# Rounded-and-rest products for the tokens' mean squares, and an earlier softmax division, in a fused attention and feed-forward kernel

## The chip, the cores and the metric

The kernel runs on one core of one Trainium2 chip. The metric is device time in microseconds (us) of one execution. The comparison is between the kernel before and the same kernel with the change below.

## What is computed

The reference has three stages, in float32.

```python
# attention, per batch (8) and head (8); 576 tokens, head width 64, 32 packing rows
p_packed = softmax(p k^T / 8) v          # first softmax, 32 rows
out      = softmax(q p_packed^T / 8) p_packed   # second softmax, 576 rows of 32 entries
x = out, heads side by side              # 4608 tokens x 512
# first feed-forward, inner width 1536
rms = sqrt(mean(x * x) + 1e-6)           # one number per token
xn  = x / rms * rms_g
x   = (silu(xn @ w_gate) * (xn @ w_val)) @ w_out
# second feed-forward
out = ((x @ w1) * (x @ w2)) @ w3 @ w_out2
```

## The kernel before, in words

**The attention is never multiplied out.** Per batch, the second softmax gives weights a2 of 32 entries per head and token. The kernel folds `p_packed`, the gain and `w_gate`/`w_val` into small matrices M (item "M" below), so that the first feed-forward's inner product is M against a2. The tokens' mean squares come from the same weights: with G the 32x32 inner products of a head's packed rows, a token's sum of squares is the sum over heads of a2^T G a2. G stands on the diagonal of two 128x128 matrices, the tile `gram` (one for even heads, one for odd: "parities"). Item "Z" multiplies `gram` by a2 on TensorE (L782); VectorE multiplies that by a2 again (L1363); GpSimd adds the parities (L648); item "SS" transposes and VectorE sums (L1368); GpSimd takes the power -0.5 (L655); after a trip through DRAM a2 is scaled by the result (L662), and a2 is split for the next batch's products.

**Rounded parts and rests.** The large products are done as three products of type fp32r: with a value x cut to x_hi (rounded, written as fp32r) and x_lo = x - x_hi, the product is hi hi + hi lo + lo hi, summed in PSUM. ScalarE (ACT) makes the hi parts and VectorE (DVE) the lo parts. The small items (S1, S2, G, Z, M, and transposes) take plain fp32 operands.

**The slots.** The main loop has 8 batches of 24 slots. A slot n handles one chunk of 128 inner columns for half the batch's tokens (288). TensorE (PE) issues in slot n:

- `into`: 12 fp32r products of 288 columns (L853 to L855), six for gate, six for val. The gate part waits for `u_ready` of slot n-1, the val part for `h_ready` of slot n-1, since they rewrite those PSUM banks (0 and 1);
- `outof`: 6 fp32r products of 512 columns (L877 to L879) from the chunk two slots earlier. It waits for `hl_ready` of the chunk;
- then the items that a table written out by hand, `SLOT_ITEMS`, puts behind this slot. They prepare the next batch (or, for S1, the one after).

ACT in slot n: the evictions of the items of slot n-1; exp1/exp2 where due; tanh of the gate part (L1262, waits for `gate_done`); the rounding of h into `g_hx` (L1269, "cast", waits for h); in even slots the issue of a small DMA (`store_rest`, L1243). DVE in slot n: the evictions of the items of slot n-1; `g_s` (L1566, waits for tanh), then `u_ready`; `g_h` (L1572), then `h_ready`; steps of the second softmax where due; "hl", the rest of h (L1587, waits for the cast), then `hl_ready`; further steps where due. Each engine takes its instructions strictly in the order written, so a wait holds all that is behind it.

The items around the change:

```python
SLOT_ITEMS = {..., 13: [("S2", 1, 1), ("M", 1, 0)], 14: [("Z", 1, 0)],
              15: [("S1", 2, 0), ("M", 1, 1)], 17: [("Z", 1, 1)], 18: [("SS", 1, 0)], ...}
```

Some items ("on gate": the first item of a slot that has two, so S2 in slot 13 and S1 in slot 15) use banks 0 and 1, the banks of gate and val. Before such an item PE waits for `u_ready` and `h_ready` of this very slot, and the next slot's gate part waits until the first half of the item has been evicted (for S2: the transposition L1357, on DVE, signal `s2_half`).

```python
for it in slot_items(n - 1):
    if on_gate(it) and it[0] in ("S1", "S2") and which == 0:
        pe.wait_ge((s1_half, s2_half)[it[0] == "S2"], 2 * it[1] + it[2] + 1)
```

The steps of the second softmax, for the two halves of the tokens (part 0 and 1): `shift2` (L1411, L1413) in slots 9 and 14; exp2 (L1131, ACT) in 11 and 15; `sums2` (L1419, L1421, L1423) in 11 and 15, behind hl; `normalize2` (L1428 and the transposition into `a2T`, L1434) in 13 and 16, between g_h and hl; `inner` writes `gram` (L1388) in slot 10; Z in 14 and 17. The S2 of part 1 writes over `a2`, so L1357 waits for the `a2T` of part 0.

Of the kernel before, what the change touches and what calls it, by code (L numbers as in the profile page):

```python
# [5 lines left out]
ALU = mybir.AluOpType  # L6
ACT = mybir.ActivationFunctionType
AX = mybir.AxisListType
F32 = mybir.dt.float32
F32R = mybir.dt.float32r  # L10

P = 128
# [51 lines left out]


SHIFT1, EXP1, SUMS1 = 21, (0, 3), 4
SHIFT2, EXP2, SUMS2, NORM2 = (9, 14), (11, 15), (11, 15), (13, 16)
GRAM = 10

REST_AHEAD = (0, 3)  # L70
WARM = 7
# [66 lines left out]
def build(nc, kT_d, qT_d, v_d, pT_d, g_d, w_gate, w_val, w_o, w12, w3T, w_out, out, r_dram, y_dram, wf_dram, rest_dram, w12_dram):  # L138
    ctx = ExitStack()
    with ctx:  # L140
        def sem(name):
            return ctx.enter_context(nc.semaphore(name))
# [21 lines left out]
        with ExitStack() as st:  # L164
            at = alloc(st)
            w_in = [at(f"w_in{i}", [P, KC, BANK]) for i in range(W_BUFS)]
            kT = at("kT", [P, HC, S])
            qT = [at(f"qT{i}", [P, HC, HALF]) for i in range(2)]
            v_sb = at("v_sb", [P, BLOCKS, HC * DH])
            pT = at("pT", [P, HC * NP])  # L170
            sc = at("sc", [P, 2, S])
            a1T = at("a1T", [P, BLOCKS * P])
            pp = at("pp", [P, 2 * DH])
            ppT = at("ppT", [P, P])
            ppTg = at("ppTg", [P, P])
            gc, gram = at("gc", [P, 2, NP]), at("gram", [P, 2, P])
            a2 = at("a2", [P, 2, HALF])
            wz = at("wz", [P, 2, HALF])
            wsum = at("wsum", [P, S])
            r_sb = at("r_sb", [P, S])  # L180
            a2T = at("a2T", [P, 2, 2, HALF])

            g_s, g_h = at("g_s", [P, HALF]), at("g_h", [P, HALF])
        w_raw, w_lo, w_hi = [None] * PAIRS, [None] * PAIRS, [None] * PAIRS

        def raw_and_lo(stack, name, shape):
# [138 lines left out]
        xy_full, xy_free = sem("xy_full"), sem("xy_free")  # L325
        nmax1_ready, bias1_ready, e1_ready = sem("nmax1_ready"), sem("bias1_ready"), sem("e1_ready")
        den1_ready, rden1_ready = sem("den1_ready"), sem("rden1_ready")
        gram_ready, s1_half, s2_half = sem("gram_ready"), sem("s1_half"), sem("s2_half")
        ppg_ready, ssum_ready, msum_ready = sem("ppg_ready"), sem("ssum_ready"), sem("msum_ready")
        max2_ready, d2_ready, e2_ready, sum2_ready = sem("max2_ready"), sem("d2_ready"), sem("e2_ready"), sem("sum2_ready")  # L330
# [37 lines left out]
        def full(eng, kind, a, part):  # L368

            eng.wait_ge(xy_full, number[kind, a, part] + 1)  # L370
# [354 lines left out]
        def _(pe):  # L725
            def item(kind, a, part):
# [44 lines left out]
                if kind == "S2":  # L771
                    freed(pe, "PT", a, 0)
                    pe.wait_ge(q_loaded[part], 16 * (a + 1))
                    for c in range(HC):
                        for par in range(2):
                            rows, cols = slice(DH * par, DH * (par + 1)), slice(NP * c, NP * (c + 1))
                            last = nc.tensor.matmul(xy[par][cols, 0:HALF], ppT[rows, cols], qT[part][rows, c, :], start=True, stop=True)
                if kind == "Z":
                    pe.wait_ge(gram_ready, a + 1)
                    pe.wait_ge(a2T_ready, 2 * a + part + 1)  # L780
                    for par in range(2):
                        last = nc.tensor.matmul(xy[par][:, 0:HALF], gram[:, par, :], a2T[:, part, par, :], start=True, stop=True)  # L782
# [303 lines left out]
        def _(act):  # L1086
# [42 lines left out]
            def exp2(a, t):  # L1129
                act.wait_ge(d2_ready, 2 * a + t + 1)  # L1130
                nc.scalar.activation(a2[:], a2[:], ACT.Exp, scale=SCALE).then_inc(e2_ready, 1)  # L1131

            def a2_split(a, t):
                act.wait_ge(a2s_ready, 2 * a + t + 1)
                if a:

                    act.wait_ge(val_done, SLOTS * a - 1 + t)
                nc.scalar.copy(a2_hi[:, t, :, :], a2T[:, t, :, :]).then_inc(a2hi_ready, 1)
# [8 lines left out]
            def wo_split(f):  # L1147
                act.wait_ge(wo_loaded[next(i for i, rows in enumerate(WO_LOADS) if f < rows.stop)], 16)
                nc.scalar.copy(wo_hi[:, f, :], wo_raw[:, f, :]).then_inc(wo_hi_ready, 1)
# [95 lines left out]
            for n in range(LAST):  # L1245
                b, s = divmod(n, SLOTS)
                f, t = divmod(s, 2)
                k = n // 2
                if s == 1 and b > 0:
                    evict(b - 1, (0, 1))  # L1250
                if s == 2 and b > 0:
                    evict(b - 1, (2,))
                for it in slot_items(n - 1):
                    item(*it)
                if b + 1 < B and s in EXP1 and n:
                    exp1(b + 1, EXP1.index(s))
                if b + 1 < B and s in EXP2:
                    exp2(b + 1, EXP2.index(s))
                act.wait_ge(gate_done, n + 1)
                if n:  # L1260
                    act.wait_ge(h_ready, n)
                nc.scalar.activation(g_s[:], in_ps[0], ACT.Tanh, scale=0.5).then_inc(s_ready, 1)  # L1262
                if n == 1:
                    wo_split(0)
                act.wait_ge(h_ready, n + 1)
                if t == 1 and k >= 2:

                    act.wait_ge(rest_stored[k % 2], 16 * (k // 2))
                nc.scalar.copy(g_hx[f % 2][:, 0, HALF * t:HALF * (t + 1)], g_h[:]).then_inc(hh_ready, 1)  # L1269
                if 0 < n < SLOTS and t == 0:  # L1270
                    wo_split(f)
                if b + 1 < B and s >= SLOTS - 2:
                    a2_split(b + 1, t)
                if t == 0 and k >= 1:
                    store_rest(k - 1)
# [73 lines left out]
        def _(dve):  # L1349
# [75 lines left out]
            def normalize2(a, t):  # L1425
                k = 2 * a + t
                dve.wait_ge(rden2_ready, k + 1)
                nc.vector.tensor_tensor(heads(a2[:]), heads(a2[:]), rden2[:].unsqueeze(2).to_broadcast([P, GROUPS2, NP]),  # L1428
                                        ALU.mult).then_inc(a2_ready, 1)
                dve.wait_ge(a2_ready, k + 1)  # L1430
                if a:

                    dve.wait_ge(a2lo_ready, k - 1)
                nc.vector.transpose(a2T[:, t, :, :], a2[:]).then_inc(a2T_ready, 1)  # L1434

            def a2_split(a, t):
                dve.wait_ge(a2hi_ready, 2 * a + t + 1)
                nc.vector.tensor_tensor(a2_lo[:, t, :, :], a2T[:, t, :, :], a2_hi[:, t, :, :].bitcast(F32),
                                        ALU.subtract).then_inc(a2lo_ready, 1)
# [116 lines left out]
            for n in range(LAST):  # L1556
                b, s = divmod(n, SLOTS)
                f, t = divmod(s, 2)
                if s == 2 and b > 0:
                    evict(b - 1)  # L1560
                behind = [it for it in slot_items(n - 1) if it[0] == "M" and it[2] not in REST_AHEAD]
                for it in slot_items(n - 1):
                    if it not in behind:
                        item(*it)
                dve.wait_ge(s_ready, n + 1)
                nc.vector.scalar_tensor_tensor(out=g_s[:], in0=g_s[:], scalar=1.0, in1=in_ps[0],  # L1566
                                               op0=ALU.add, op1=ALU.mult).then_inc(u_ready, 1)
                dve.wait_ge(u_ready, n + 1)
                dve.wait_ge(val_done, n + 1)
                if n:  # L1570
                    dve.wait_ge(hl_ready, n)
                nc.vector.scalar_tensor_tensor(out=g_h[:], in0=g_s[:], scalar=0.5, in1=in_ps[1],  # L1572
                                               op0=ALU.mult, op1=ALU.mult).then_inc(h_ready, 1)
                if n == 1:
                    wo_split(0)
                if b + 1 < B and s == SUMS1:
                    sums1(b + 1)
                if b + 1 < B and s in SHIFT2:
                    shift2(b + 1, SHIFT2.index(s))
                if b + 1 < B and s in NORM2:  # L1580
                    normalize2(b + 1, NORM2.index(s))
                for it in behind:
                    if n > 1:
                        item(*it)
                dve.wait_ge(hh_ready, n + 1)
                own = slice(HALF * t, HALF * (t + 1))
                nc.vector.tensor_tensor(g_hx[f % 2][:, 1, own], g_h[:], g_hx[f % 2][:, 0, own].bitcast(F32),  # L1587
                                        ALU.subtract).then_inc(hl_ready, 1)
                if n == 1:

                    item("M", 0, 2)
                if 0 < n < SLOTS and t == 0:
                    wo_split(f)
                if b + 2 < B and s == SHIFT1:
                    shift1(b + 2)
                if b + 1 < B and s == GRAM:
                    inner(b + 1)
                if b + 1 < B and s in SUMS2:
                    sums2(b + 1, SUMS2.index(s))
                if b + 1 < B and s >= SLOTS - 2:  # L1600
                    a2_split(b + 1, t)
            for c in range(FC):
# [152 lines left out]
```

## Time and profile before

| what | value |
|---|---|
| median of 3 runs | 1320.36 us (1319.73 to 1320.95) |
| the profiled execution: its own time | 1319.28 us |
| the profiled execution: span, first to last instruction | 1317.7 us |
| PE busy | 1311.3 us, 100% of the span |
| DVE busy | 874.2 us, 66% |
| ACT busy | 411.8 us, 31% |
| POOL busy | 122.4 us, 9% |
| chain that ended last | PE 98%, DVE 1% |
| main loop of 192 slots | from 61.2 us to about 736 us |

The busy share of PE is of records that overlap: a product of 288 columns shows 0.29 us, while the next one starts 0.13 us after it. What a product costs is read from start to start. "PEld" rows are weight loads, which run beside the product before. On DVE and ACT too an instruction can start up to 0.1 us before the one ahead is shown as ended, when nothing makes it wait. A timeline row has the start, the duration, the engine, the line and operation, output and inputs with their shapes, and in brackets the idle time before it with the engine that ended the idle time.

### The profile page before, as it was taken

The numbers are of one execution on the slowest core, as the hardware profiler recorded it, in microseconds if no ns is written. First come the engines' busy times: TensorE is split into PE (matmuls) and PEld (weight loads), VectorE is DVE, ScalarE is ACT, GpSimd is POOL, SyncE is SP. The second block draws the span as 40 slices with busy tenths as digits, with TensorE's granted clock in tenths as the row PEclk, the third lists the DMA queues.
The fourth block names the chain that finished last, engine by engine and source line by source line (L and its number), as shares of the span: only waits on it lengthen the run. The fifth ranks groups of instructions, "written<-read, shape, count | busy, mean of one in ns | idle before, by whom it ended". The sixth has DMA issues, their size and how long they took to land.

```text
span 1317.7 us, 21671 instructions
## 1 busy us (share of the span) xinstructions
PE 1311.3 (100%) x8590; PEld 1089.4 (83%) x8590; DVE 874.2 (66%) x1373; ACT 411.8 (31%) x787; POOL 122.4 (9%) x92
## 2 busy tenths in 40 slices
PE   9999999999999999999999999999999999999998
PEld 7788878888878888887888899888888888888887
DVE  5668667576565765756754677866766686677666
ACT  5344433434434344343333433311200120112000
POOL 0100101001000010010100531100200010020000
PEclk9999999999999999999999999999999999999999
DMA  9773435343534434333426386845454335545301
GB/s 356 245 271 121 158 123 168 127 160 108 173 97 159 167 118 162 125 120 104 114 77 234 139 312 264 308 142 183 128 176 160 128 117 195 179 147 188 101 1 64
DMA packets 117202, 211.40 MB, mean 160 GB/s; under 512 B 33904, under 2 KB 35952, under 8 KB 114032
## 3 DMA queue, kind: packets, MB, share of 16 engines
q1 hardware_dynamic: 90672, 203.21, 45.0%
q10 hardware_dynamic: 26432, 6.82, 2.3%
q8 instruction: 69, 1.13, 0.4%
q14 instruction: 29, 0.24, 0.1%
HBM read 168.04 MB, written 41.96 MB: 159 GB/s over the span
## 4 chain that ended last, share of the span: by engine, by line
PE 98%; DVE 1%; ACT 0%; DMA 0%; issue 0%; SPq 0%; ACTq 0%
PE psum L965 9%; PE psum L967 9%; PE psum L966 9%; PE psum L853 8%; PE psum L855 8%; PE psum L854 8%; PE psum L879 7%; PE psum L878 7%; PE psum L877 7%; PE psum L1008 4%; PE psum L1010 4%; PE psum L1009 4%; PE psum L798 3%; PE psum L819 1%; PE psum L782 1%; PE psum L824 1%
## 5 line engine op out<-in xcount | busy, mean ns | idle before, releaser
L853 PE MATMUL psum<-a_hi,m_hi 128*128 128x288 f32 x768 | 235.2, 306 | 1.2 <-DVE g_s L1566 0.4
L855 PE MATMUL psum<-a_hi,m_lo 128*128 128x288 f32 x768 | 226.4, 295 | 0.0
L854 PE MATMUL psum<-a_lo,m_hi 128*128 128x288 f32 x768 | 226.2, 295 | 0.0
L853 PEld LDWEIGHTS psum<-a_hi,m_hi 128*128 128x128 f32 x768 | 144.2, 188 | 47.1 <-issue 39.6
L1566 DVE SCALAR_TENSOR_TENSOR g_s<-g_s,psum 128x288 f32<-128x288 f32 x192 | 86.6, 451 | 129.7 <-ACT g_s L1262 129.1
L879 PE MATMUL psum<-g_hx,wo_lo 128*128 128x512 f32 x384 | 152.3, 397 | 0.0
L878 PE MATMUL psum<-g_hx,wo_hi 128*128 128x512 f32 x384 | 151.6, 395 | 0.0
L1269 ACT CAST g_hx<-g_h 128x288 fp32r<-128x288 f32 x192 | 83.1, 433 | 218.5 <-DVE g_h L1572 215.5
L877 PE MATMUL psum<-g_hx,wo_hi 128*128 128x512 f32 x384 | 150.3, 391 | 0.0
L854 PEld LDWEIGHTS psum<-a_lo,m_hi 128*128 128x128 f32 x768 | 144.4, 188 | 5.2
L855 PEld LDWEIGHTS psum<-a_hi,m_lo 128*128 128x128 f32 x768 | 144.1, 188 | 0.0
L1587 DVE TENSOR_TENSOR g_hx<-g_h,g_hx 128x288 fp32r<-128x288 f32 x192 | 90.2, 470 | 68.6 <-ACT g_hx L1269 68.6
L1340 ACT CAST hhd<-hd_raw 128x1024 fp32r<-128x1024 f32 x15 | 15.8, 1054 | 295.7 <-DVE hd_raw L1680 286.8
L1262 ACT ACTIVATE g_s<-psum 128x288 f32<-128x288 f32 x192 | 78.9, 411 | 93.1 <-PE psum L855 91.6
L1008 PE MATMUL psum<-wf_hi,hhd 128*128 128x512 f32 x256 | 100.4, 392 | 0.1
L1010 PE MATMUL psum<-wf_hi,hd_lo 128*128 128x512 f32 x256 | 99.7, 389 | 0.0
L1009 PE MATMUL psum<-wf_lo,hhd 128*128 128x512 f32 x256 | 99.7, 389 | 0.0
L1514 DVE TENSOR_TENSOR bd<-bd,psum 128x512 f32<-128x512 f32 x96 | 65.8, 687 | 41.1 <-PE psum L1010 39.9
L1572 DVE SCALAR_TENSOR_TENSOR g_h<-g_s,psum 128x288 f32<-128x288 f32 x192 | 87.1, 454 | 6.9 <-DVE g_s L1566 0.3
L965 PE MATMUL psum<-xd_hi,w_hi 128*128 128x512 f32 x224 | 87.2, 389 | 0.0
L966 PE MATMUL psum<-xd_lo,w_hi 128*128 128x512 f32 x224 | 87.2, 389 | 0.0
L967 PE MATMUL psum<-xd_hi,w_lo 128*128 128x512 f32 x224 | 87.1, 389 | 0.0
(188 smaller groups left out, 2413.9 us busy)
## 6 DMA issues: line engine op xcount, KB each, us to landing
w_in<-in_w_gate SPq DMA_DIRECT2D x24, 1024.0 KB, 7.3
w_in<-in_w_val SPq DMA_DIRECT2D x24, 1024.0 KB, 5.2
wb_hi<-w_scratch SPq DMA_DIRECT2D x56, 256.0 KB, 2.8
wb_lo<-w_scratch SPq DMA_DIRECT2D x56, 256.0 KB, 3.1
w_hi<-w_scratch SPq DMA_DIRECT2D x49, 256.0 KB, 3.0
w_lo<-w_scratch SPq DMA_DIRECT2D x49, 256.0 KB, 3.9
kT<-in_kT SPq DMA_DIRECT2D x8, 1152.0 KB, 7.2
v_sb<-in_v SPq DMA_DIRECT2D x8, 1152.0 KB, 9.9
```

The source lines that it names most:

```text
L853: nc.tensor.matmul(in_ps[which], hi, a2_hi[:, t, par, :], start=par == 0, stop=False)
L854: nc.tensor.matmul(in_ps[which], hi, a2_lo[:, t, par, :], start=False, stop=False)
L855: last = nc.tensor.matmul(in_ps[which], lo, a2_hi[:, t, par, :], start=False, stop=par == 1)
L877: nc.tensor.matmul(out_ps[m], hi, hh, start=f == 0, stop=False)
L878: nc.tensor.matmul(out_ps[m], hi, hl, start=False, stop=False)
L879: last = nc.tensor.matmul(out_ps[m], lo, hh, start=False, stop=f == FC - 1)
L965: nc.tensor.matmul(dst, hi, xhi[:, c, :], start=c == 0, stop=False)
L966: nc.tensor.matmul(dst, hi, xlo[:, c, :], start=False, stop=False)
L967: last = nc.tensor.matmul(dst, lo, xhi[:, c, :], start=False, stop=c == 1)
L1008: nc.tensor.matmul(dst, hhd[:, f, cols], wf_hi[:, chunk, :], start=f == 1, stop=False)
L1009: nc.tensor.matmul(dst, hhd[:, f, cols], wf_lo[:, chunk, :], start=False, stop=False)
L1010: last = nc.tensor.matmul(dst, hld[:, f, cols], wf_hi[:, chunk, :], start=False, stop=f == 0)
```

## The change

The Z of batches 1 to 7 no longer multiplies `gram` by `a2T` in fp32, but takes three fp32r products per parity from four new tiles: `gram_hi`, `gram_lo`, `z_hi`, `z_lo`. Batch 0, whose preparation is ahead of the loop, keeps the fp32 products. ACT makes `gram_hi` in slot 11 and `z_hi` in slots 12 and 16, each behind the slot's cast; DVE makes `gram_lo` in slot 11, behind hl and ahead of `sums2`, and `z_lo` in slots 13 and 16, as the last step of the slot. `normalize2` of part 0 goes from slot 13 to slot 12 (same place, between g_h and hl); that of part 1 goes from slot 16, between g_h and hl, to slot 15, behind `sums2`. Z stays in slots 14 and 17.

```diff
-SHIFT2, EXP2, SUMS2, NORM2 = (9, 14), (11, 15), (11, 15), (13, 16)
+SHIFT2, EXP2, SUMS2, NORM2 = (9, 14), (11, 15), (11, 15), 12
 GRAM = 10
+GRAM_SPLIT, Z_HI, Z_LO = 11, (12, 16), (13, 16)
...
+            gram_hi, gram_lo = at("gram_hi", [P, 2, P], F32R), at("gram_lo", [P, 2, P], F32R)
+            z_hi, z_lo = at("z_hi", [P, 2, HALF], F32R), at("z_lo", [P, 2, HALF], F32R)
...
-                if kind == "Z":
+                if kind == "Z" and a:
+                    pe.wait_ge(z_lo_ready, 3 * (a - 1) + part + 2)
+                    for par in range(2):
+                        nc.tensor.matmul(xy[par][:, 0:HALF], gram_hi[:, par, :], z_hi[:, par, :], start=True, stop=False)
+                        nc.tensor.matmul(xy[par][:, 0:HALF], gram_hi[:, par, :], z_lo[:, par, :], start=False, stop=False)
+                        last = nc.tensor.matmul(xy[par][:, 0:HALF], gram_lo[:, par, :], z_hi[:, par, :], start=False, stop=True)
+                if kind == "Z" and a == 0:
                     pe.wait_ge(gram_ready, a + 1)
                     pe.wait_ge(a2T_ready, 2 * a + part + 1)
...
(ACT)
+            def gram_split(a):
+                act.wait_ge(gram_ready, a + 1)
+                if a > 1:
+                    full(act, "Z", a - 1, 1)
+                nc.scalar.copy(gram_hi[:], gram[:]).then_inc(z_hi_ready, 1)
+            def z_split(a, t):
+                act.wait_ge(a2T_ready, 2 * a + t + 1)
+                if t:
+                    full(act, "Z", a, 0)
+                nc.scalar.copy(z_hi[:], a2T[:, t, :, :]).then_inc(z_hi_ready, 1)
...
                 nc.scalar.copy(g_hx[f % 2][:, 0, HALF * t:HALF * (t + 1)], g_h[:]).then_inc(hh_ready, 1)
                 if 0 < n < SLOTS and t == 0:
                     wo_split(f)
+                if b + 1 < B and s == GRAM_SPLIT:
+                    gram_split(b + 1)
+                if b + 1 < B and s in Z_HI:
+                    z_split(b + 1, Z_HI.index(s))
...
(DVE)
+            def gram_split(a):
+                dve.wait_ge(z_hi_ready, 3 * (a - 1) + 1)
+                if a > 1:
+                    full(dve, "Z", a - 1, 1)
+                nc.vector.tensor_tensor(gram_lo[:], gram[:], gram_hi[:].bitcast(F32), ALU.subtract).then_inc(z_lo_ready, 1)
+            def z_split(a, t):
+                dve.wait_ge(z_hi_ready, 3 * (a - 1) + t + 2)
+                if t:
+                    full(dve, "Z", a, 0)
+                nc.vector.tensor_tensor(z_lo[:], a2T[:, t, :, :], z_hi[:].bitcast(F32), ALU.subtract).then_inc(z_lo_ready, 1)
...
-                if b + 1 < B and s in NORM2:
-                    normalize2(b + 1, NORM2.index(s))
+                if b + 1 < B and s == NORM2:
+                    normalize2(b + 1, 0)
...
                 if b + 1 < B and s == GRAM:
                     inner(b + 1)
+                if b + 1 < B and s == GRAM_SPLIT:
+                    gram_split(b + 1)
                 if b + 1 < B and s in SUMS2:
                     sums2(b + 1, SUMS2.index(s))
+                if b + 1 < B and s == SUMS2[1]:
+                    normalize2(b + 1, 1)
+                if b + 1 < B and s in Z_LO:
+                    z_split(b + 1, Z_LO.index(s))
                 if b + 1 < B and s >= SLOTS - 2:
                     a2_split(b + 1, t)
```

## Rows read from the trace of the kernel before

**Rows 1.** The page: the chain that ended last, by engine.

```profile
PE 98%; DVE 1%; ACT 0%; DMA 0%; issue 0%; SPq 0%; ACTq 0%
```

**Rows 2.** Timeline of PE: end of slot 11, start of slot 12.

```profile
188.81 0.40 PE L879 MATMUL psum<-g_hx,wo_lo 128*128 128x512 f32 x1
189.04 0.29 PE L853 MATMUL psum<-a_hi,m_hi 128*128 128x288 f32 x1
189.17 0.29 PE L854 MATMUL psum<-a_lo,m_hi 128*128 128x288 f32 x1
```

**Rows 3.** Timeline of PE: end of slot 14 with its Z, start of slot 15.

```profile
199.59 0.40 PE L879 MATMUL psum<-g_hx,wo_lo 128*128 128x512 f32 x1
199.82 1.14 PE L782 MATMUL psum<-a2T,gram 128*128 128x288 f32 x4
...
200.92 0.29 PE L854 MATMUL psum<-a_lo,m_hi 128*128 128x288 f32 x1
```

**Rows 4.** Instructions on the tile a2T (ns min/median/max): the subtraction for a2_lo.

```profile
L1438 DVE TENSOR_TENSOR a_lo<-a2T,a_hi x16: 754/759/1272, 58.8 to 661.7; 128x576 fp32r<-128x576 f32 x16
```

**Rows 5.** Timeline of PE: end of slot 13, its items, start of slot 14.

```profile
194.77 0.40 PE L879 MATMUL psum<-g_hx,wo_lo 128*128 128x512 f32 x1
195.09 0.71 PE L777 MATMUL psum<-qT,ppT 64*32 64x288 f32 x16
195.60 1.06 PE L798 MATMUL psum<-w_in,ppTg 64*32 64x512 f32 x16
196.76 0.37 PE L853 MATMUL psum<-a_hi,m_hi 128*128 128x288 f32 x1
196.97 0.29 PE L854 MATMUL psum<-a_lo,m_hi 128*128 128x288 f32 x1
```

**Rows 6.** Timeline of PE: M of slot 15, start of slot 16.

```profile
204.38 1.06 PE L798 MATMUL psum<-w_in,ppTg 64*32 64x512 f32 x16
...
205.61 0.30 PE L854 MATMUL psum<-a_lo,m_hi 128*128 128x288 f32 x1
```

**Rows 7.** Timeline of DVE: hl of slot 11 to the eviction of S2 in slot 14.

```profile
188.94 0.46 DVE L1587 TENSOR_TENSOR g_hx<-g_h,g_hx 128x288 fp32r<-128x288 f32 x1 [0.50 <-ACT g_hx L1269]
189.31 0.75 DVE L1419 TENSOR_REDUCE sum<-a 128x18 f32<-128x576 f32 x1
...
190.49 0.44 DVE L1566 SCALAR_TENSOR_TENSOR g_s<-g_s,psum 128x288 f32<-128x288 f32 x1
190.96 0.45 DVE L1572 SCALAR_TENSOR_TENSOR g_h<-g_s,psum 128x288 f32<-128x288 f32 x1
191.92 0.46 DVE L1587 TENSOR_TENSOR g_hx<-g_h,g_hx 128x288 fp32r<-128x288 f32 x1 [0.50 <-ACT g_hx L1269]
193.45 0.46 DVE L1566 SCALAR_TENSOR_TENSOR g_s<-g_s,psum 128x288 f32<-128x288 f32 x1 [1.08 <-ACT g_s L1262]
...
194.31 0.75 DVE L1428 TENSOR_TENSOR a<-a,rden 128x576 f32<-128x576 f32 x1
195.10 0.78 DVE L1434 STREAM_TRANSPOSE a2T<-a 128x576 f32<-128x576 f32 x1
...
196.14 0.47 DVE L1357 STREAM_TRANSPOSE a<-psum 128x288 f32<-128x288 f32 x1
```

**Rows 8.** Timeline of ACT: cast of slot 11, tanh of slot 13; then slot 23.

```profile
188.47 0.43 ACT L1269 CAST g_hx<-g_h 128x288 fp32r<-128x288 f32 x1 [1.01 <-DVE g_h L1572]
...
193.01 0.41 ACT L1262 ACTIVATE g_s<-psum 128x288 f32<-128x288 f32 x1 [1.12 <-PE psum L855]
...
232.80 0.67 ACT L1138 CAST a_hi<-a2T 128x576 fp32r<-128x576 f32 x1
233.38 0.20 ACT L1122 ACTIVATE bias<-nmax 128x2 f32<-128x2 f32 x1
```

**Rows 9.** Timeline of DVE: hl of slot 15, g_s of slot 16.

```profile
203.84 0.46 DVE L1587 TENSOR_TENSOR g_hx<-g_h,g_hx 128x288 fp32r<-128x288 f32 x1 [0.50 <-ACT g_hx L1269]
...
206.91 0.45 DVE L1566 SCALAR_TENSOR_TENSOR g_s<-g_s,psum 128x288 f32<-128x288 f32 x1 [1.44 <-ACT g_s L1262]
```

More of the change, by code:

```diff
@@ L327, in build @@
         den1_ready, rden1_ready = sem("den1_ready"), sem("rden1_ready")
+        z_hi_ready, z_lo_ready = sem("z_hi_ready"), sem("z_lo_ready")
         gram_ready, s1_half, s2_half = sem("gram_ready"), sem("s1_half"), sem("s2_half")
```

## The prediction, made before the changed kernel ran

> **What bounds the kernel now.** I read the page first. TensorE (PE) is busy for the whole span, and the chain that ended last is PE for 98% of it [rows 1]. So work on ACT or DVE costs nothing while it stays beside PE, and every stop of PE is paid in full. The question is what PE saves in Z, and whether what ACT and DVE get to do makes PE wait. The second view is therefore PE's timeline, start to start, since the records overlap. Without items, the last `outof` product of a slot starts at 188.81 and the second `into` product of the next slot at 189.17, 0.36 us later; the first begins the slot at 189.04 [rows 2]. The third view is the timelines of DVE and ACT in slots 11 to 16, read for how much time lies between the moment a signal is given and the moment PE wants it. All times below are of one batch; the slots repeat in the others.
>
> One place is already tight. From the start of M in slot 13 to the second product of slot 14 it is 196.97 - 195.60 = 1.37 us [rows 5]; behind the M of slot 15 it is 205.61 - 204.38 = 1.23 [rows 6]. The missing 0.14 us is a wait: slot 14's gate part needs S2's first half evicted, and that transposition starts at 196.14 [rows 7], 0.62 us ahead of PE's product at 196.76 [rows 5]. DVE, not PE, sets the start of slot 14 now, and whatever makes DVE later there makes the kernel longer.
>
> **What Z gives back.** With Z between, the last `outof` product and the second `into` product are 200.92 - 199.59 = 1.33 us apart [rows 3], against 0.36 without: Z costs 0.97 us. After the change it is six fp32r products of 288 columns, like those of `into`. The first product of slot 12 starts 0.23 us after the last `outof` one and the second 0.13 later [rows 2]. So six cost 0.13 to 0.133 each, 0.80 us at most, and the gain is 0.17 to 0.18 us for each Z. Changed are 7 batches of two parts: 14 x 0.175 = 2.45 us. A Z is recorded as four instructions [rows 3], two for each of its two fp32 products, at 0.97 / 4 = 0.24 each. Bounds per Z: nothing gained if products from the new tiles step more slowly than in `into`, 0.24 gained if each of the six took half of such a record.
>
> Rows give 0.97 for two fp32 products, 0.24 per record. The Trainium skill, page FP8 and Floating Point Precision, section TensorE Precision Notes, says that true fp32 takes four passes through the array; three passes against four would be a quarter of 0.97 saved, 0.24 per Z and 3.4 us in all, an estimate by that page. The trace agrees only in part: fp32r products step at 0.13 [rows 2], not at 0.12, a quarter of one fp32 product.
>
> **What the moves cost: the chain into slot 14.** I follow it from hl of slot 11, start 188.94, which the change leaves where it is.
>
> - ACT: `gram_hi` starts behind the cast of slot 11 (188.47 [rows 8]), at about 188.8, and lasts under 0.43, what the cast of 288 columns takes. DVE's `gram_lo` can start at about 189.3, where hl leaves DVE free (188.94 to 189.31 [rows 7]). For 256 columns it holds DVE about 0.34, a little under hl's 0.37.
> - `sums2` therefore starts at 189.65, not 189.31. It holds DVE for 1.18 (189.31 to 190.49), so g_s of slot 12 starts at 190.82, g_h 0.47 later (190.49 to 190.96) at 191.29. PE wants them at about 192.0 and 192.8 (slot 12 began at 189.04 [rows 2]; a slot without items is 12 x 0.13 + 6 x 0.23, about 3.0): no stop here.
> - New in slot 12: `normalize2`. It starts 0.37 after g_h, at 191.66; its transposition 0.79 later (194.31 to 195.10 [rows 7]), at 192.45, takes 0.78.
> - ACT waits for that: `z_hi` at about 193.26, 0.03 after the transposition ends, as g_s starts 0.03 after tanh ends (193.01 + 0.41 to 193.45 [rows 7, 8]). Behind it on ACT stands tanh of slot 13, which ran at 193.01 before [rows 8]. A rounding of this size lets the next ACT instruction start 0.58 later (232.80 to 233.38 [rows 8]): tanh at 193.84. The DMA that ACT issues in slot 12 stands behind `z_hi` as well, goes out beside it about 1.8 us later than now, and its data is first read after the loop. tanh is 0.83 late.
> - g_s of slot 13 follows tanh by 0.44 (193.01 to 193.45 [rows 7]): 194.28. g_h 0.48 later, 194.77, ends at 195.22. S2, which started at 195.09 [rows 5], waits for it: it starts about 0.2 late. hl follows g_h by 0.96 (190.96 to 191.92): 195.73.
> - New in slot 13: `z_lo` of part 0, at 196.10. The same subtraction takes 0.76 [rows 4] and, like hl, lets the next start 0.08 or 0.09 before its end: 0.67 to 0.68. S2's eviction starts at 196.77 or 196.78 instead of 196.14.
> - PE follows 0.62 later, at 197.40 instead of 196.76.
>
> Slot 14 starts 0.64 us late, S2's own lateness included. That `normalize2` left slot 13 gives DVE 1.49 us there, but the wait on tanh, `gram_lo` and `z_lo` take more. **Bounds of this stop.** Low: 0.57, if S2's eviction counts from its end by the shortest hand-over of these rows (0.03 after the end of a 0.47 us instruction, and as much for PE's load) instead of the 0.62. High: 0.80, if the new hand-over of `a2T` and one other show the tail of 0.15 that PE shows behind S2's eviction (0.62 - 0.47). I take 0.64, to which every step has a row of its own kind.
>
> **Is anything else late?** M's eviction, shift2 and exp2 move with PE. Slot 15 starts 0.64 - 0.17 = 0.47 late. There DVE gets `normalize2` of part 1 behind `sums2`. hl of slot 15, 203.84 before [rows 9], comes at about 204.2 to 204.3; `sums2` 1.18 and the division and transposition (about 0.1 of own wait, 0.79, and 0.78 less the usual 0.08) end at about 207.4. g_s of slot 16 was at 206.91 [rows 9] and would be at 207.4 with PE: DVE is free just as it is due, and PE wants that signal only at the start of slot 17, over 1 us later. In slot 16 1.49 us leave DVE and 0.67 (`z_lo`) come. `z_hi` of part 1 finds its input ready. In slot 17 Z finds `z_lo` over 1 us old, and in slot 14 over 3 us. Hidden at no price: `gram_hi`, `z_hi` of part 1, `z_lo` of part 1. If PE did not lead there, `z_lo` would cost its 0.67 us per batch. No step on POOL or on SP's queue is moved; what they wait for (Z's eviction, M's products) moves with PE.
>
> **The sum.** Per batch: 0.64 lost in slot 13, 2 x 0.175 = 0.35 saved: 0.29 us longer. Seven batches: +2.0 us. The profiled execution took 1319.28 us (span 1317.7), so it would take 1321.3. That execution is 1.1 below the median 1320.36 of the runs; against the median the forecast is 1322.4 us, +0.15%. A difference under 0.2%, 2.6 us, is about what a measurement of this kernel can't tell from none.
>
> **Rivals.**
>
> 1. *The chain hands over more slowly (slower).* Place: `a2T` to `z_hi` to tanh of slot 13. The trace has no engine waiting for `a2T` at once. For: PE's product came 0.15 behind the end of S2's transposition. Against: the one hand-over from ACT to DVE in the rows takes 0.03. It decides slower if the stop passes 0.35 + 0.38 = 0.73 us per batch. At 0.8 to 0.9 it is +3.1 to +3.9 us: 1323.5 to 1324.3. Chance 0.22.
> 2. *The chain is not binding (only the gain).* `z_hi` would have to cost tanh nothing. For: PE stands well ahead of DVE elsewhere. Against: slot 14 already starts on S2's eviction [rows 5 to 7]; `z_lo` alone, put ahead of it, is 0.67. It gives 1320.4 - 2.4 = 1317.9. Chance 0.08.
> 3. *Z becomes no cheaper.* If the weights of six short products are not hidden here, Z takes 0.97 as before (the change then doesn't do what it says) and only the stop is left: 7 x 0.64 = +4.5, 1324.9. Against: `into` loads the same kind of weights beside products of the same width. Chance 0.05.
> 4. *A second stop in slots 16 or 17*, where DVE is just free at 207.4. It must be over 0.6 us late to reach PE; then 0.1 to 0.4 us per batch on top, 1323.1 to 1325.2. Chance 0.07.
>
> The forecast has the rest, 0.58. With the gain per Z from 0.15 to 0.20 and the stop from 0.57 to 0.75, it goes from +1.2 to +3.2: 1321.5 to 1323.6.
>
> **How the numbers follow.** Of the forecast's 0.58 about 0.13 lies above +2.6 us; with rival 1 (0.19 of it), rival 3 (0.05) and rival 4 (0.06) slower has 0.43. Rival 2 straddles -2.6 us and gives faster 0.04; two more hundredths go to a gain near the page's figure together with it: 0.06. The rest, 0.51, is no change. The range holds the forecast, rival 1 and rival 4 and leaves out most of rivals 2 and 3: 1319.8 to 1325.6, with 0.6 us of the runs' own spread at either end.
>
> **What would show it.** In the changed profile: Z as six products at 0.13, the distance of 1.33 become 1.16. `z_hi` of slot 12 starts right after `a2T`, and tanh of slot 13 right after `z_hi`, released by ACT's own order and not by PE. S2's eviction behind `z_lo`, and from the last `outof` product of slot 13 to the start of slot 14 about 2.6 us in place of 196.76 - 194.77 = 1.99 [rows 5], with PE idle ahead of S2 and ahead of slot 14. No new idle time on PE in slots 15 to 18. I am wrong if slot 13 is not longer, if tanh of slot 13 still starts 1.0 us into its slot, or if another slot has grown.

## The result, and the profile after

| kernel | median | runs |
|---|---|---|
| before | 1320.95 us (1319.18 to 1321.94) | 9 |
| changed | 1323.25 us (1322.65 to 1324.57) | 9 |

The ratio is 1.0022, with a 95% interval of 1.0014 to 1.0030: 1.8 to 4.0 us slower, where 2.0 was forecast; the two medians are 2.3 us apart. The profiled execution of the changed kernel took 1322.82 us, with a span of 1321.2 and a granted clock of 1.000.

The chain that ended last, by engine (page of the changed kernel; compare [rows 1]):

```profile
PE 93%; DVE 4%; ACT 1%; issue 1%; POOL 0%; ACTq 0%; POOLq 0%
```

DVE and ACT now hold 5% of the chain between them; before it was 1% [rows 1]. The waits of PE and of its weight loads say where (engine and line waited for: us in total, times, longest; two views of the changed kernel):

```profile
PE psum L865 <- DVE a L1385: 3.4, 7, 0.5
```

```profile
PEld psum L783 <- DVE g_s L1606: 4.4, 7, 0.9
```

L865 is the first gate product of a slot, L1385 the eviction of S2, L783 S2 itself: seven waits of each kind, one per batch. The second view puts S2's wait down to the line of g_s; the g_h behind it is the later of the two signals that S2 waits for.

Timeline of PE in the changed kernel, the same batch as [rows 5] (the whole batch lies 0.9 us later): the end of slot 13, S2, M and the start of slot 14.

```profile
195.68 0.40 PE L891 MATMUL psum<-g_hx,wo_lo 128*128 128x512 f32 x1
196.25 0.72 PE L783 MATMUL psum<-qT,ppT 64*32 64x288 f32 x16 [0.17 <-issue]
196.73 1.09 PE L810 MATMUL psum<-w_in,ppTg 64*32 64x512 f32 x16
198.31 0.37 PE L865 MATMUL psum<-a_hi,m_hi 128*128 128x288 f32 x1 [0.48 <-DVE a L1385]
```

From the last `outof` product to slot 14 it is 198.31 - 195.68 = 2.63 us, against 1.99 before; "about 2.6" was forecast. S2 starts 0.57 behind that product in place of 0.32, and slot 14 starts 1.58 behind M in place of 1.16.

The chain behind that, on DVE, hl of slot 11 to S2's eviction (compare [rows 7]):

```profile
189.85 0.46 DVE L1627 TENSOR_TENSOR g_hx<-g_h,g_hx 128x288 fp32r<-128x288 f32 x1 [0.50 <-ACT g_hx L1293]
190.23 0.42 DVE L1468 TENSOR_TENSOR gram_lo<-gram,gram_hi 128x256 fp32r<-128x256 f32 x1
190.56 0.75 DVE L1447 TENSOR_REDUCE sum<-a 128x18 f32<-128x576 f32 x1
...
191.74 0.40 DVE L1606 SCALAR_TENSOR_TENSOR g_s<-g_s,psum 128x288 f32<-128x288 f32 x1
192.17 0.45 DVE L1612 SCALAR_TENSOR_TENSOR g_h<-g_s,psum 128x288 f32<-128x288 f32 x1
192.54 0.75 DVE L1456 TENSOR_TENSOR a<-a,rden 128x576 f32<-128x576 f32 x1
193.32 0.78 DVE L1462 STREAM_TRANSPOSE a2T<-a 128x576 f32<-128x576 f32 x1
194.03 0.41 DVE L1627 TENSOR_TENSOR g_hx<-g_h,g_hx 128x288 fp32r<-128x288 f32 x1
195.21 0.45 DVE L1606 SCALAR_TENSOR_TENSOR g_s<-g_s,psum 128x288 f32<-128x288 f32 x1 [0.77 <-ACT g_s L1286]
195.69 0.45 DVE L1612 SCALAR_TENSOR_TENSOR g_h<-g_s,psum 128x288 f32<-128x288 f32 x1
196.65 0.46 DVE L1627 TENSOR_TENSOR g_hx<-g_h,g_hx 128x288 fp32r<-128x288 f32 x1 [0.50 <-ACT g_hx L1293]
197.02 0.75 DVE L1474 TENSOR_TENSOR z_lo<-a2T,z_hi 128x576 fp32r<-128x576 f32 x1
197.69 0.47 DVE L1385 STREAM_TRANSPOSE a<-psum 128x288 f32<-128x288 f32 x1
```

and on ACT, `gram_hi` in slot 11, then `z_hi` and tanh of slot 13 (compare [rows 8]):

```profile
189.72 0.40 ACT L1149 CAST gram_hi<-gram 128x256 fp32r<-128x256 f32 x1
190.94 0.41 ACT L1286 ACTIVATE g_s<-psum 128x288 f32<-128x288 f32 x1 [0.82 <-PE psum L867]
192.65 0.43 ACT L1293 CAST g_hx<-g_h 128x288 fp32r<-128x288 f32 x1 [1.30 <-DVE g_h L1612]
194.13 0.67 ACT L1155 CAST z_hi<-a2T 128x576 fp32r<-128x576 f32 x1 [1.05 <-DVE a2T L1462]
194.14 0.52 ACTq L1267 DMA_DIRECT2D rest_scratch<-g_hx  x1
194.76 0.41 ACT L1286 ACTIVATE g_s<-psum 128x288 f32<-128x288 f32 x1
```

ACT's `z_hi` waits for `a2T` (L1462), with the DMA issue beside it, and tanh of slot 13 starts only at 194.76, 1.82 us into a slot that began at 192.94; it was 0.99 before. From hl of slot 11 to S2's eviction 7.84 us pass; before it was 196.14 - 188.94 = 7.20.

Z in slot 14, with the products around it (compare [rows 3]):

```profile
201.14 0.40 PE L891 MATMUL psum<-g_hx,wo_lo 128*128 128x512 f32 x1
201.38 0.29 PE L787 MATMUL psum<-z_hi,gram_hi 128*128 128x288 f32 x1
201.51 0.29 PE L788 MATMUL psum<-z_lo,gram_hi 128*128 128x288 f32 x1
201.64 0.29 PE L789 MATMUL psum<-z_hi,gram_lo 128*128 128x288 f32 x1
201.77 0.29 PE L787 MATMUL psum<-z_hi,gram_hi 128*128 128x288 f32 x1
201.90 0.30 PE L788 MATMUL psum<-z_lo,gram_hi 128*128 128x288 f32 x1
202.03 0.29 PE L789 MATMUL psum<-z_hi,gram_lo 128*128 128x288 f32 x1
202.16 0.29 PE L865 MATMUL psum<-a_hi,m_hi 128*128 128x288 f32 x1
202.30 0.29 PE L866 MATMUL psum<-a_lo,m_hi 128*128 128x288 f32 x1
```

Last `outof` product to second `into` product: 202.30 - 201.14 = 1.16 us, against 1.33. Z costs 0.80 in place of 0.97.

The start of one slot to the start of the next, read off PE's timeline for every batch, gives the whole account. All slots not listed are equal within 0.1 us, but for slots 22, 23 and 0 of some batches and slot 2 of batch 0, of which more below. Slots 14 and 15, and 17 and 18, stand together because a slot's first product is recorded 0.34 us ahead of the second behind the fp32 Z (200.58 and 200.92 in the kernel before) and 0.14 ahead behind the fp32r Z (202.16 and 202.30): the border between two slots moves, their sum doesn't.

| slots | before, batches 0 to 6 | changed, batches 1 to 6 | changed, batch 0 |
|---|---|---|---|
| 13 (S2, M) | 4.73 to 4.74 | 5.37 to 5.38 | 5.69 |
| 14 and 15 (Z; S1, M) | 8.61 (8.69 in batch 0, 8.13 in 6) | 8.44 (7.96 in 6) | 8.43 |
| 17 and 18 (Z; SS) | 7.51 (7.48 in batch 6) | 7.34 | 7.34 |

### The profile page after: what moved, and what is told of

The parts are those of the page before. It is cut to its first block, busy times and chain, and to the rows that moved or that the text cites. A ratio compares the mean times of both kernels' runs of the same rounds, so it can differ in the third digit from the quotient of the medians.

```text
span 1321.2 us, 21795 instructions
## 1 busy us (share of the span) xinstructions
PE 1310.8 (99%) x8618; PEld 1090.9 (83%) x8618; DVE 887.7 (67%) x1394; ACT 422.3 (32%) x808; POOL 121.5 (9%) x92
## 4 chain that ended last, share of the span: by engine, by line
PE 93%; DVE 4%; ACT 1%; issue 1%; POOL 0%; ACTq 0%; POOLq 0%
PE psum L977 9%; PE psum L979 9%; PE psum L978 9%; PE psum L865 8%; PE psum L867 7%; PE psum L866 7%; PE psum L891 6%; PE psum L890 6%; PE psum L889 6%; PE psum L1020 4%; PE psum L1022 4%; PE psum L1021 4%; PE psum L810 3%; PE psum L831 1%; PE psum L836 1%; PE psum L841 1%
## 5 line engine op out<-in xcount | busy, mean ns | idle before, releaser
L865 PE MATMUL psum<-a_hi,m_hi 128*128 128x288 f32 x768 | 232.8, 303 | 3.8 <-DVE a L1385 3.4
L865 PEld LDWEIGHTS psum<-a_hi,m_hi 128*128 128x128 f32 x768 | 144.2, 188 | 49.7 <-issue 43.0
L1627 DVE TENSOR_TENSOR g_hx<-g_h,g_hx 128x288 fp32r<-128x288 f32 x192 | 91.5, 477 | 68.3 <-ACT g_hx L1293 68.3
```

Source lines behind the costliest of these rows:

```text
L865: nc.tensor.matmul(in_ps[which], hi, a2_hi[:, t, par, :], start=par == 0, stop=False)
```

## The experiments

Distances of slots are read as in the table above. Medians and ratios are against the kernel before, run beside each on the same chip.

**1. The division alone.** The kernel before, with only this changed:

```diff
-SHIFT2, EXP2, SUMS2, NORM2 = (9, 14), (11, 15), (11, 15), (13, 16)
+SHIFT2, EXP2, SUMS2, NORM2 = (9, 14), (11, 15), (11, 15), 12
...
-                if b + 1 < B and s in NORM2:
-                    normalize2(b + 1, NORM2.index(s))
+                if b + 1 < B and s == NORM2:
+                    normalize2(b + 1, 0)
...
+                if b + 1 < B and s == SUMS2[1]:
+                    normalize2(b + 1, 1)
```

> The kernel before with only the two divisions moved (slot 13 to 12, slot 16 to behind the sums of slot 15); Z stays fp32, no splits. Theory (tanh of slot 13 is late only because z_hi stands before it and waits for a2T; z_lo stands before S2's eviction): nothing waits for the earlier division, DVE is free earlier in slot 13, so S2's eviction starts as soon as PE is through with S2, and slot 13 shrinks from 4.74 to about 4.6 us; 7 x 0.15 = 1.0 us faster than before, about 1319.9. Rival A (the moved division itself makes DVE late): slot 13 grows by up to 0.64, +4.5 us.

Measured: 1319.42 us against 1320.72, ratio 0.9990 (0.9981 to 0.9999). Slot 13 is 4.57 to 4.58 in all seven batches. Rival A falls: the earlier division by itself takes away what slot 14 already waited for S2's eviction. From the start of slot 13 to the second product of slot 14 it is 4.81 us in place of 4.95, so the wait was 0.14; the first product alone shows 0.16, since without a wait it is recorded 0.24 ahead of the second and with one 0.21. (The same 0.03 stands in slot 13 of experiments 3 and 6.) The stop comes from the splits around it.

**2. The stop without the gain.** The changed kernel with `gram` and `a2T` in Z again, splits and waits kept:

```diff
                     pe.wait_ge(z_lo_ready, 3 * (a - 1) + part + 2)
                     for par in range(2):
-                        nc.tensor.matmul(xy[par][:, 0:HALF], gram_hi[:, par, :], z_hi[:, par, :], start=True, stop=False)
-                        nc.tensor.matmul(xy[par][:, 0:HALF], gram_hi[:, par, :], z_lo[:, par, :], start=False, stop=False)
-                        last = nc.tensor.matmul(xy[par][:, 0:HALF], gram_lo[:, par, :], z_hi[:, par, :], start=False, stop=True)
+                        last = nc.tensor.matmul(xy[par][:, 0:HALF], gram[:, par, :], a2T[:, part, par, :], start=True, stop=True)
```

> The changed kernel with all splits and waits kept, but Z of every batch in fp32 from gram and a2T. Isolates the cost of the stop from the gain. Theory: slot 13 stays at 5.38, each of 14 Z costs 0.97 again in place of 0.80: 2.4 us slower than the changed kernel, 4.8 us slower than before (0.36%). Rival B (fp32r products gain nothing net, since PE only waits elsewhere for what it saved): no slower than the changed kernel, within 0.5 us.

Measured: 1325.05 us against 1320.72, ratio 1.0033 (1.0020 to 1.0045), 4.3 us slower. Slot 13 is 5.37 to 5.38 (5.68 in batch 0), slots 14 and 15 together 8.60, slots 17 and 18 together 7.51. The distances show stop and gain independent of each other: 14 x 0.17 = 2.4 us are lost again, as forecast, and the loops of the two profiles are 2.6 us apart. The medians of the time show less: those of this kernel and of the changed one are 1.8 us apart, were measured on different occasions, and the intervals of the two ratios overlap, so the time alone doesn't settle the size of the gain. Rival B, which allowed 0.5, falls by the distances.

**3. `z_lo` of part 0 behind S2's eviction.**

```diff
-GRAM_SPLIT, Z_HI, Z_LO = 11, (12, 16), (13, 16)
+GRAM_SPLIT, Z_HI, Z_LO = 11, (12, 16), (None, 16)
...
                     if it not in behind:
                         item(*it)
+                    if it[0] == "S2" and it[2] == 1:
+                        z_split(it[1], 0)
```

> The changed kernel with z_lo of part 0 put in slot 14 between the evictions of S2 and M, where DVE waits for M's rounding anyway. Theory: S2's eviction starts 0.67 earlier, then M's own products set the start of slot 14, 0.99 after M's start; slot 13 about 4.78 in place of 5.38; 7 x 0.6 = 4.2 us faster than the changed kernel, 2.1 faster than before. Rival C (the tanh of slot 13 is the only thing that matters, z_lo has slack): no change to the changed kernel.

Measured: 1320.07 us against 1320.72, ratio 0.9999 (0.9990 to 1.0008): about 3 us faster than the changed kernel (ratios 0.9999 and 1.0022, forecast 4.2), but not the 2.1 faster than before: the interval of the time reaches from 1.3 us faster to 1.1 slower. Slot 13 is 4.82 (5.13 in batch 0). The 0.56 us came back, so rival C falls; what stays, 0.25 above the 4.57 of experiment 1, is S2's own wait for the late g_h. The rest of the miss is batch 0 (0.3 in slot 13; 0.4 in slot 15, for which see experiment 6; 0.4 in slots 1 to 3, which stays open) and 0.9 us in slots 22, 23 and 0 around the ends of batches 1 and 2 in the profiled execution.

**4. `z_hi` of part 0 behind the cast of slot 13**, `z_lo` where the change has it:

```diff
-GRAM_SPLIT, Z_HI, Z_LO = 11, (12, 16), (13, 16)
+GRAM_SPLIT, Z_HI, Z_LO = 11, (13, 16), (13, 16)
```

> The changed kernel with only z_hi of part 0 moved from slot 12 to slot 13, behind the cast; z_lo stays at the end of slot 13, ahead of S2's eviction. Theory: tanh of slot 13 is on time (1.0 us into its slot), z_lo starts when z_hi is through, S2's eviction 0.62 earlier than in the changed kernel; slot 13 about 4.75; 4.3 us faster than the changed kernel, 2.1 to 2.4 faster than before. If instead the delay of tanh cost nothing: slot 13 stays at 5.38.

Measured: 1319.53 us against 1321.29, ratio 0.9986 (0.9977 to 0.9995). That is 1.8 us faster than before (0.7 to 3.0) where 2.1 to 2.4 was forecast. Slot 13 is 4.74 to 4.76 in batches 1 to 6, as forecast. In batch 0 it is 5.64, and only 0.05 came back: DVE splits `wo` in slot 12 as well, so g_s of slot 13 comes only 0.23 us earlier behind hl of slot 11, though tanh is on time; and `z_lo`, which stood 0.38 behind hl of slot 13, stands 0.57 behind it, since `z_hi` now waits for the cast.

**5. `gram_lo` one slot later:**

```diff
-                if b + 1 < B and s == GRAM_SPLIT:
+                if b + 1 < B and s == GRAM_SPLIT + 1:
                     gram_split(b + 1)
                 if b + 1 < B and s in SUMS2:
```

> The changed kernel with gram_lo moved from slot 11, ahead of the sums, to slot 12 behind hl. Theory: the whole chain (sums, g_s, g_h, division, transposition, z_hi, tanh) comes 0.33 earlier: slot 13 about 5.05 in place of 5.38, 2.3 us faster than the changed kernel, the time of the kernel before. If gram_lo was hidden: no change.

Measured: 1321.73 us against 1321.29, ratio 1.0000 (0.9990 to 1.0010). Slot 13 is 5.10 to 5.11 in five of seven batches (5.48 in batch 0; 5.39 in batch 2, where DVE stood 0.31 us between g_s and g_h of slot 12 for a reason that stays open; the kernel before has the same pause once, in slot 11 of batch 3). `gram_lo`'s 0.33 us was 0.27 of the stop.

**6. Both splits of part 0 late** (the edits of experiments 3 and 4, with `Z_HI, Z_LO = (13, 16), (None, 16)`):

> As z_lo_late, and z_hi of part 0 put in slot 13 behind the cast, so that tanh of slot 13 no longer waits for it. Theory: PE meets no wait in slot 13; 4.6 us in place of 5.38 (and of 4.74 before); Z keeps its gain: 3.4 to 3.5 us faster than before (0.26%), 5.8 faster than the changed kernel. Rival D (more work on ACT and DVE costs as such, wherever it stands): at most half of that.

Measured: 1318.14 us against 1320.72, ratio 0.9982 (0.9974 to 0.9991). Slot 13 is 4.57 to 4.58 (4.87 in batch 0), slots 14 and 15 together 8.46, slots 17 and 18 together 7.34. DVE and PE there, two views of this kernel:

```profile
196.21 0.48 DVE L1385 STREAM_TRANSPOSE a<-psum 128x288 f32<-128x288 f32 x1 [0.56 <-PE psum L783]
196.61 0.44 DVE L1386 STREAM_TRANSPOSE a<-psum 128x288 f32<-128x288 f32 x1
196.98 0.71 DVE L1474 TENSOR_TENSOR z_lo<-a2T,z_hi 128x576 fp32r<-128x576 f32 x1
198.11 1.23 DVE L1407 TENSOR_TENSOR m_lo<-psum,m_hi 128x1024 fp32r<-128x1024 f32 x1 [0.42 <-ACT m_hi L1127]
```

```profile
195.38 0.72 PE L783 MATMUL psum<-qT,ppT 64*32 64x288 f32 x16
195.89 1.06 PE L810 MATMUL psum<-w_in,ppTg 64*32 64x512 f32 x16
196.88 0.40 PE L865 MATMUL psum<-a_hi,m_hi 128*128 128x288 f32 x1
```

S2's eviction waits for PE (0.56 us idle, put down to L783), not PE for it; `z_lo` stands in time in which DVE waits for M's rounding, and 0.42 of that is still idle. This version is faster than both kernels: 2.6 us less than before, 5.1 less than the changed one, by medians measured on different occasions. The forecast was 3.4 to 3.5. Of the miss 0.3 us lie in slot 13 of batch 0 and 0.4 in its slot 15 (4.96 in place of 4.59), which is a stop at another place: in batch 0 DVE has a split of `wo` (L1492) in slot 14 too, works without a pause from 113.31 to 117.69, and g_s of slot 15 is the last of that work. S1 waits for g_s and g_h (DVE, then the weight loads of PE):

```profile
115.98 0.69 DVE L1492 TENSOR_TENSOR wo_lo<-wo_raw,wo_hi 128x512 fp32r<-128x512 f32 x1
...
117.25 0.44 DVE L1608 SCALAR_TENSOR_TENSOR g_s<-g_s,psum 128x288 f32<-128x288 f32 x1
```

```profile
118.25 0.21 PEld L743 LDWEIGHTS psum<-kT,pT 64*32 64x32 f32 x16 [0.71 <-DVE g_s L1608]
```

In the later batches no S1 waits for DVE. Rival D allowed 1.75 us at most; the interval of the time reaches from 1.2 to 3.4 us and doesn't exclude that by itself, but the distances do: in batches 1 to 6 slots 13 to 18 keep the whole gain, and all else that is lost there is 0.2 us around the end of batch 3.

**7. GpSimd's scaling halved**, to explain subtractions of unusual length (see the last section). The odd parity of `a2T` is left unscaled:

```diff
-                nc.gpsimd.tensor_tensor(a2T[:, t, :, :], a2T[:, t, :, :],
-                                        r_sb[:, HALF * t:HALF * (t + 1)].unsqueeze(1).to_broadcast([P, 2, HALF]),
-                                        ALU.mult).then_inc(a2s_ready, 1)
+                nc.gpsimd.tensor_tensor(a2T[:, t, 0, :], a2T[:, t, 0, :],
+                                        r_sb[:, HALF * t:HALF * (t + 1)], ALU.mult).then_inc(a2s_ready, 1)
```

> The changed kernel with GpSimd's scaling of a2T cut to the even parity (the odd half stays unscaled), so each of its two instructions is about half as long (0.7 in place of 1.44 us). It is to tell why single hl subtractions on DVE took 1.0 to 1.7 us in place of 0.46 where they began beside that scaling. If a DVE subtraction is held until the GpSimd instruction ends, the longest hl of the loop falls to 1.1 us or less; if it is another cause, hl of 1.4 us and more remain.

Measured: 1324.71 us in its one run, slot 13 as in the changed kernel. The longest hl of the loop is 1.00 us, against 1.73, 1.53 and 1.40 in the changed kernel, and against a longest one of 1.41 to 1.67 in each of the seven other kernels that scale both parities.

## Why the prediction was right, and where it was off

**What bounds the kernel, and the tight place: right.** Slot 14 waited for S2's eviction already before; experiment 1 shows the wait's size, 0.14 us as it was read, by removing it.

**The gain per Z: right.** 0.175 was forecast, 0.17 to 0.18 measured, in all 14 Z (8.61 to 8.44 and 7.51 to 7.34), and experiment 2 loses it again. The Trainium skill (page FP8 and Floating Point Precision, section TensorE Precision Notes) has four passes for fp32; the estimate from it, three passes in place of four, would have made the gain 0.24, but the distances decide against that size.

**The chain into slot 14: right step by step in six of seven batches.** Forecast against measured, from hl of slot 11: `sums2` +0.71 and +0.71; g_h of slot 12 +2.35 and +2.32; `a2T` +3.51 and +3.47; `z_hi` +4.32 and +4.28; tanh of slot 13 +4.90 and +4.91; `z_lo` +7.16 and +7.17; S2's eviction +7.83 or +7.84 and +7.84; PE 0.62 behind it, both. The stop was 0.64 and is 0.64. Experiments 3, 4 and 5 take single terms out, and the stop shrinks by 0.56, 0.62 and 0.27. The two bounds of the stop do not come out as they are written: 0.03 + 0.47 + 0.03 in place of 0.62 gives 0.55 and not 0.57, and a tail of 0.15 in place of 0.03 at two hand-overs gives 0.88 and not 0.80. The stop lies inside either pair.

**The term that was mis-sized: "seven batches" at the same price.** Batch 0 loses 5.69 - 4.74 = 0.95 us, not 0.64. What the prediction had wrong is "the slots repeat in the others": the chain does not start equally far ahead of slot 13 in every batch. In batch 0 DVE also splits `wo` in the even slots. The split in slot 10 makes g_s of slot 11 start 1.75 us into its slot in place of 1.43, and hl of slot 11 comes later by as much, as these rows of the changed kernel show (DVE, then PE at the start of slot 13):

```profile
103.59 0.46 DVE L1627 TENSOR_TENSOR g_hx<-g_h,g_hx 128x288 fp32r<-128x288 f32 x1 [0.50 <-ACT g_hx L1293]
```

```profile
106.36 0.29 PE L865 MATMUL psum<-a_hi,m_hi 128*128 128x288 f32 x1
```

That is 2.77 us ahead, against 192.94 - 189.85 = 3.09 in batch 1: the 0.32 us that are missing. The kernel before has the same 2.77 us in batch 0, but there the late hl cost nothing: slot 13 was 4.74 as elsewhere. In the changed kernel S2's eviction stands 7.84 us behind that hl in batch 0 as in batch 1, so all of its lateness reaches PE. With it the stop is 6 x 0.64 + 0.95 = 4.8 us against 7 x 0.64 = 4.5, and the balance with 14 Z is +2.3 us.

**Slots 15 to 17: right.** `a2T` of part 1 and g_s of slot 16 (DVE, changed kernel; compare [rows 9]):

```profile
207.51 0.78 DVE L1462 STREAM_TRANSPOSE a2T<-a 128x576 f32<-128x576 f32 x1
208.29 0.45 DVE L1606 SCALAR_TENSOR_TENSOR g_s<-g_s,psum 128x288 f32<-128x288 f32 x1
```

DVE is free at 208.29, just as g_s has been due since 208.26 (tanh ended 207.85 + 0.41), and PE shows no wait. `z_lo` of part 1 and `gram_hi` cost nothing.

**The rivals.** None came: the hand-overs were those of the rows (1), the stop is there (2), Z is cheaper (3), and there is no second stop of PE in slots 16 or 17 (4). The measured 0.22% lies just beyond the 0.2% that was called the limit of no change, on the side of rival 1, yet by batch 0 and by what follows here, not by slower hand-overs. With an interval of 0.16% in all, that limit was wider than it had to be.

**What is left.** The profiled spans are 3.5 us apart, 1321.2 and 1317.7. Of this 0.5 lie ahead of the loop, which starts at 61.71 and 61.17; in the kernels of the experiments it starts between 61.37 and 62.38, in no order of what they change. From the first slot to the start of the last one the loop is 675.25 us in the changed kernel (736.96 - 61.71) and 672.28 before: +2.97, of which +2.3 are the balance above. In this execution 0.7 us lie in slots 22, 23 and 0 around the ends of batches 2 and 4, slot 0 of batch 1 is 0.3 shorter than before, and slots 2 and 3 of batch 0 are 0.2 longer; such slots differ from kernel to kernel and batch to batch without a pattern in the change. The mechanism of slots 22 and 23 of batch 2 is in the last section; how much of the 2.3 us between the medians such stops make is open, since only one execution of each is profiled. So the mechanism was forecast, but that the time came out so near 2.0 is partly luck: batch 0 was not in the sum, nor were these stops.

## What to carry to other kernels

A step that is moved ahead takes with it the wait of whatever is put behind it: the earlier division was a gain, but a rounding that waits for it was put ahead of the next tanh on an engine that takes its work in order. Put a split behind the time-critical instructions of its slot, or into a gap in which its engine waits for something else anyway, and look for the consumer's deadline and not for the earliest time that its input is there. Before multiplying a stop by the number of batches, read the first batch too: its engines may have other work in the same slots.

## What was not expected of the hardware

**A DVE subtraction is held while GpSimd works on SBUF.** Timelines of the changed kernel, behind slot 21 of batch 2: GpSimd's two scalings of `a2T`, and DVE's hl with what follows.

```profile
314.02 3.03 POOL L668 TENSOR_TENSOR a2T<-a2T,r_sb 128x576 f32<-128x576 f32 x2 [7.52 <-DMA r_sb<-r_scratch]
```

```profile
314.04 1.73 DVE L1627 TENSOR_TENSOR g_hx<-g_h,g_hx 128x288 fp32r<-128x288 f32 x1 [0.50 <-ACT g_hx L1293]
315.69 1.34 DVE L1425 TENSOR_REDUCE nmax<-sc 128x2 f32<-128x1152 f32 x1
316.96 0.44 DVE L1606 SCALAR_TENSOR_TENSOR g_s<-g_s,psum 128x288 f32<-128x288 f32 x1
```

hl takes 1.73 us in place of 0.46 and ends at 315.77. One scaling takes 1.44 us (below), so the first ends at about 315.5: hl ends about 0.3 us after it. The other two long hl of this kernel began 0.21 and 0.36 us into the first scaling of their batch, took 1.53 and 1.40, and ended 0.30 and 0.32 behind it by the same count. g_s of slot 22 starts at 316.96, behind a reduction that was pushed back too, and PE starts slot 23 0.33 us late. The reduction itself ran beside the second scaling without being held: it takes 1.34 or 1.35 us in every batch. The instructions of L668 and L1627 in the changed kernel, and of L668 in the kernel with the scaling halved (ns min/median/max):

```profile
L668 POOL TENSOR_TENSOR a2T<-a2T,r_sb x16: 1426/1439/1711, 56.3 to 659.9; 128x576 f32<-128x576 f32 x16
```

```profile
L1627 DVE TENSOR_TENSOR g_hx<-g_h,g_hx x192: 415/458/1730, 65.0 to 739.8; 128x288 fp32r<-128x288 f32 x192
```

```profile
L668 POOL TENSOR_TENSOR a2T<-a2T,r_sb x16: 806/810/1026, 57.1 to 659.8; 128x288 f32<-128x288 f32 x16
```

With scalings of 0.81 us the longest hl is 1.00. It stands here (GpSimd, then DVE, halved scaling):

```profile
573.22 1.57 POOL L668 TENSOR_TENSOR a2T<-a2T,r_sb 128x288 f32<-128x288 f32 x2 [6.65 <-DMA r_sb<-r_scratch]
```

```profile
574.10 1.00 DVE L1626 TENSOR_TENSOR g_hx<-g_h,g_hx 128x288 fp32r<-128x288 f32 x1 [0.50 <-ACT g_hx L1292]
```

The second scaling runs from about 574.0 to 574.8, hl ends at 575.10, again 0.3 us behind. So a long instruction on GpSimd sets how long DVE's subtraction stands. The Trainium skill, page SBUF — State Buffer, section Who interferes with whom, has the rule: a DVE instruction with two SBUF inputs and a GpSimd instruction that reads SBUF contend for the port pair that the two engines share, the pair is locked exclusively, and the order of issue decides who is blocked. The trace agrees for hl (two SBUF inputs, up to 1.73 us) and for the reduction (one input, not held). When the scaling begins depends on a trip of the norms through DRAM (it waits 7 us for it), so the collisions fall elsewhere in each profiled kernel, the one before included (hl of 1.41 us at 655.22), and a few tenths of a us of PE's time go or stay with them. Whether the whole of the 0.3 us behind the scaling is hl's own work was not tried.
